# A fused attention and two-MLP kernel: early steps in another order on three engines, and the low parts of x on another engine

## The reference

```python
scores = where(causal, -1e9, q @ k.T / 8); a = softmax(scores)
local = a @ v
mem_out = (phi(q) @ M_prev) / (phi(q) @ z_prev + 1e-6)      # phi(x) = elu(x) + 1
x = g * mem_out + (1 - g) * local                           # g = sigmoid(beta), one per head
h = x @ w_in                                                # 2304 x 512 @ 512 x 1024
solu = h * softmax(h); ln = (solu - mu) / sqrt(var + 1e-6) * g_ln; x = ln @ w_out
return (sigmoid(x @ w_gate) * (x @ w_val)) @ w_out2         # 1536 wide
```

## Time and profile before

| | |
|---|---|
| median of 3 runs | 845.45 us |
| the profiled execution | 845.53 us |
| its span, first to last instruction | 843.5 us |
| PE busy over the span | 816.5 us, 97% |
| DVE, ACT, POOL busy | 601.1, 466.3, 39.0 us |
| mean granted TensorE clock | 0.995 of full |
| early steps (scores of step 1 to those of step 5) | 14.3 to 64.2 us |
| steps with the first MLP's tiles | 64.2 to 338.6 us |
| last tiles of the first MLP | 338.6 to 411 us |

### The profile page before, as it was taken

The page is one execution under the profiler, slowest core; times in us unless marked ns, Lnnn a source line. Parts: engine busy times, 40 slices in busy tenths (PEclk is TensorE's granted clock), DMA queues, the critical chain, the costliest instruction groups (busy, mean ns, idle before and its releaser), DMA issues.

```text
span 843.5 us, 15401 instructions
## 1 busy us (share of the span) xinstructions
PE 816.5 (97%) x5704; PEld 686.0 (81%) x5704; DVE 601.1 (71%) x1447; ACT 466.3 (55%) x965; POOL 39.0 (5%) x47
## 2 busy tenths in 40 slices
PE   5888999999999999999999999999999999999997
PEld 3555777777777777878889999999999999999996
DVE  6988877777777775588565777687676678666653
ACT  6987666666566663364444444574444465444442
POOL 1000000000000001111000000000000000000000
PEclk8999999999999999999999999999999999999999
DMA  7353011111111000100224111103111113111002
GB/s 219 91 171 88 18 53 54 53 54 54 47 44 54 26 18 15 51 1 1 75 54 148 51 51 51 51 26 125 50 51 51 51 27 125 51 51 50 26 1 76
DMA packets 67034, 49.51 MB, mean 59 GB/s; under 512 B 9360, under 2 KB 57488, under 8 KB 66960
## 3 DMA queue, kind: packets, MB, share of 16 engines
q1 hardware_dynamic: 66960, 48.53, 19.3%
HBM read 43.79 MB, written 4.72 MB: 58 GB/s over the span
## 4 chain that ended last, share of the span: by engine, by line
PE 90%; DVE 5%; issue 2%; ACT 2%; SPq 1%; DMA 1%; POOL 0%; DVEq 0%; ACTq 0%
PE tt_bk L1554 10%; PE tt_bk L1552 10%; PE tt_bk L1553 10%; PE m_bk L1420 10%; PE s_bk L1444 7%; PE tt_bk L1349 5%; PE s_bk L1290 4%; PE o_bk L1357 4%; PE o_bk L1444 4%; PE s_bk L1604 3%; PE s_bk L1605 3%; PE s_bk L1603 3%; PE m_bk L1604 2%; PE m_bk L1605 2%; PE m_bk L1603 2%
## 5 line engine op out<-in xcount | busy, mean ns | idle before, releaser
L1554 PE MATMUL tt_bk<-xc_hi,wc_lo 128*128 128x384 f32 x476 | 160.0, 336 | 0.0
L1552 PE MATMUL tt_bk<-xc_hi,wc_hi 128*128 128x384 f32 x476 | 159.9, 336 | 0.0
L1553 PE MATMUL tt_bk<-xc_lo,wc_hi 128*128 128x384 f32 x476 | 159.8, 336 | 0.0
L588 ACT ACTIVATE p_nat<-p_nat,negmax 128x512 f32<-128x512 f32 (+2 forms) x144 | 83.0, 579 | 53.3 <-DVE negmax L905 53.3
L1133 DVE TENSOR_TENSOR wc_lo<-wc_raw,wc_hi 128x768 fp32r<-128x768 f32 x72 | 78.3, 1088 | 32.0 <-ACT wc_hi L653 32.0
L1552 PEld LDWEIGHTS tt_bk<-xc_hi,wc_hi 128*128 128x128 f32 x476 | 89.4, 188 | 6.1
L1553 PEld LDWEIGHTS tt_bk<-xc_lo,wc_hi 128*128 128x128 f32 x476 | 89.4, 188 | 6.1
L1554 PEld LDWEIGHTS tt_bk<-xc_hi,wc_lo 128*128 128x128 f32 x476 | 89.4, 188 | 0.0
L905 DVE CUSTOM_DVE_ANT_0 p_nat<-s_bk,mask 128x384 f32<-128x384 f32 (+2 forms) x124 | 54.9, 489 | 19.4 <-PE s_bk L1290 18.9
L653 ACT CAST wc_hi<-wc_raw 128x768 fp32r<-128x768 f32 x72 | 64.5, 946 | 3.1 <-DVE wc_raw L1127 3.1
L1349 PE MATMUL tt_bk<-ident,p_nat 128*128 128x128 f32 x400 | 56.6, 277 | 7.6 <-ACT pT L595 7.4
(11 more groups left out here) (215 smaller groups left out, 1781.1 us busy)
## 6 DMA issues: line engine op xcount, KB each, us to landing
wc_raw<-in_moe_w_val SPq DMA_DIRECT2D x36, 256.0 KB, 3.0
wc_raw<-in_moe_w_gate SPq DMA_DIRECT2D x36, 256.0 KB, 3.4
qkT<-in_q SPq DMA_DIRECT2D x16, 288.0 KB, 2.8
qkT<-in_k SPq DMA_DIRECT2D x16, 288.0 KB, 3.2
v_raw<-in_v SPq DMA_DIRECT2D x16, 256.0 KB, 2.7
out<-o_sb SPq DMA_DIRECT2D x15, 256.0 KB, 2.5
w_raw<-in_moe_w_out SPq DMA_DIRECT2D x12, 256.0 KB, 4.5
turned<-in_k SPq DMA_DIRECT2D x32, 72.0 KB, 2.5
```

The source lines that it names most:

```text
L588: nc.scalar.activation(p_tile(g, tile), p_tile(g, tile), ACT.Exp, bias=negmax[:, n:n + 1], scale=-1.0, accum_out=den[:, n:n + 1]).then_inc ...
L1552: mm(o, hi[:, k, c, :], xc_hi[:, j, c, :], start=start and c == 0, stop=False, skip_group_check=True)
L1553: mm(o, hi[:, k, c, :], xc_lo[:, j, c, :], start=False, stop=False, skip_group_check=True)
L1554: last = mm(o, lo[:, k, c, :], xc_hi[:, j, c, :], start=False, stop=c == 1, skip_group_check=True)
```

## The change

Seven edits, all in the order of instructions but one.

1. Early steps, ScalarE: the copies of turned weights 0 to 2 stand ahead of exponential tile 2, and copies 3 to 6 ahead of tile 4; the copies of the values' result stand apart.
2. Early steps, VectorE: `normalize(g, 0)` stands right behind unit 3, `scale_memory(g - 1, 0)` behind unit 5, and `scale_memory(g - 1, 1)` with the split of the first weight behind unit 6, `feature` last.
3. Early steps, TensorE: `weighted` is two parts, the tail part behind `scores(g, 1)`; `memory` stands behind `turn_p(g - 1, 2)`.
4. Last pair's step (g = 16): TensorE transposes the MLP's tile ahead of the values and the output tile behind them; ScalarE has `moe_ln` ahead of `keep_both`; VectorE has `moe_ln_low` between two normalisations.
5. `split_x`, the low part of x, moves from GpSimd to VectorE for the tiles 0 to 12 but 4: tile 0 behind unit 3 of step 5, the others at the end of the step before theirs.
6. GpSimd keeps tile 4, the tiles from 13 on, and `rstd`.
7. Behind the steps: `moe_ln(12)` ahead of `moe_square(13)` on ScalarE, `moe_ln_low(12)` ahead of `moe_var(13)` on VectorE, with `low_xc(0, B21)` later.

```diff
 # GpSimd
-            def step(g):
-                if g >= M0:
-                    rstd(g - M0)
-                if g >= M0 - 1:
-                    split_x(g - M0 + 1)
...
+            def step(g, t):
+                if t and t in OWN:
+                    split_x(t)
+                rstd(t)
 # ScalarE, early_step
                 if g > 1:
-                    keep_both(g - 2)
+                    keep_x(g - 2, 0)
                 if g:
                     keep_pt(g - 1, 0)
+                if g > 1:
+                    keep_x(g - 2, 1)
+                if g:
                     keep_pt(g - 1, 1)
-                for n in range(2, 6):
+                    keep_pt(g - 1, 2)
+                exp_tile(g, 2)
+                exp_tile(g, 3)
+                if g:
+                    for n in range(3, NF):
+                        keep_pt(g - 1, n)
+                for n in range(4, 6):
                     exp_tile(g, n)
-                if g:
-                    keep_pt(g - 1, 2)
-                    keep_pt(g - 1, 3)
...
                 exp_tile(g, 6)
                 exp_tile(g, 7)
-                if g:
-                    keep_pt(g - 1, 4)
-                    keep_pt(g - 1, 5)
-                    keep_pt(g - 1, 6)
 # ScalarE, step
-                if t > 1 and g < PAIRS:
+                if t > 1:
                     moe_ln(t - 1)
                 keep_both(g - 2)
-                if t == 1 or g == PAIRS:
+                if t == 1:
                     moe_ln(t - 1)
 # ScalarE, behind the steps
             moe_y(t, True)
+            moe_ln(t + 1)
             moe_square(t + 2)
 # VectorE
+            def split_x(t):
+                dve.wait_ge(x_hi_ok, t + 1)
+                nc.vector.tensor_tensor(x_lo[:, :, :], xT[:, :, bass.ds(t * P, P)],
+                                        x_hi[:, :, :].bitcast(F32), ALU.subtract).then_inc(x_lo_ok, 1)
 # VectorE, early_step
                 unit_max(g, 2)
                 unit_max(g, 3)
+                normalize(g, 0)
+                unit_max(g, 4)
+                unit_max(g, 5)
                 if g:
                     scale_memory(g - 1, 0)
+                unit_max(g, 6)
+                if g:
                     scale_memory(g - 1, 1)
                     for c in W1_LO_MEM.get(g, ()):
                         split_w1(c)
-                unit_max(g, 4)
-                unit_max(g, 5)
                 feature(g)
...
-                unit_max(g, 6)
-                normalize(g, 0)
 # VectorE, step
-                if t > 1 and g < PAIRS:
+                if t:
                     moe_ln_low(t - 1)
...
-                if t == 1 or g == PAIRS:
-                    moe_ln_low(t - 1)
...
+                if t == 0:
+                    split_x(t)
...
                 moe_norm(t)
+                if t + 1 not in OWN:
+                    split_x(t + 1)
 # VectorE, behind the steps
-            low_xc(0, B21)
+            moe_ln_low(t + 1)
             moe_var(t + 2)
             moe_norm(t + 2, False)
+            low_xc(0, B21)
 # TensorE, early_step
                 if g > 1:
-                    weighted(g - 2)
+                    weighted_main(g - 2)
                 scores(g, 1)
+                if g > 1:
+                    weighted_tail(g - 2)
                 if g:
                     turn_p(g - 1, 0)
                     turn_p(g - 1, 1)
-                    memory(g - 1, None)
                 scores(g, 2)
                 if g:
-                    for n in range(2, 5):
-                        turn_p(g - 1, n)
+                    turn_p(g - 1, 2)
+                    memory(g - 1, None)
+                    turn_p(g - 1, 3)
+                    turn_p(g - 1, 4)
                 scores(g, 3)
 # TensorE, step
-                if g == PAIRS:
-                    pe.wait_ge(u_ok, t)
-                    weighted(g - 2)
-                if t > 1:
+                if 1 < t and g < PAIRS:
                     moe_out_t(t - 2)
...
-                if g < PAIRS:
-                    weighted(g - 2)
+                weighted(g - 2)
+                if g == PAIRS:
+                    moe_out_t(t - 2)
```

More of the change, by code:

```diff
@@ L551, in rstd @@
                 nc.gpsimd.tensor_tensor(st[:, 6:7], st[:, 5:6], half[:, :], ALU.pow).then_inc(rstd_ok, 1)
-            def step(g):
-                if g >= M0:
-                    rstd(g - M0)
-                if g >= M0 - 1:
-                    split_x(g - M0 + 1)
-            for g in range(PAIRS + 1):
-                step(g)
+            def step(g, t):
+                if t and t in OWN:
+                    split_x(t)
+                rstd(t)
+            for g in range(M0, PAIRS + 1):
+                step(g, g - M0)
             split_x(T_END + 2)
@@ L842, in _ @@
                 even = (i - t) % 2 == 1
-                moe_ln(i)
+                if i > t + 1:
+                    moe_ln(i)
                 if i == t + 1:
@@ L1238, in _ @@
             moe_stats(t + 2)
-            low_xc(0, B21)
+            moe_ln_low(t + 1)
             moe_var(t + 2)
             moe_norm(t + 2, False)
+            low_xc(0, B21)
             for i in range(t + 1, TILES):
                 even = (i - t) % 2 == 1
-                moe_ln_low(i)
+                if i > t + 1:
+                    moe_ln_low(i)
                 if i + 2 >= TILES:
@@ L1362, in turn_memory, with weighted_main @@
                    is_transpose=True, skip_group_check=True)
-            def weighted(h):
+            def weighted_main(h):
                 wait(pe, x_ok, 2 * h)
@@ L1381, in weighted, with weighted_tail @@
                 last.then_inc(o_ready, 1)
+            def weighted_tail(h):
                 for j in range(ST):
@@ L1385, in weighted @@
                 last.then_inc(o_ready, 1)
+            def weighted(h):
+                weighted_main(h)
+                weighted_tail(h)
             def memory(g, t):
```

## The result

| | before | changed |
|---|---|---|
| median | 845.45 us | 852.61 us (849.87 to 852.86) |
| the profiled execution's span | 843.5 us | 850.9 us |
| mean granted TensorE clock | 0.995 | 0.988 |

The ratio is 1.0074, with a 95% interval of 1.0063 to 1.0086: 6.3 us slower. The two medians lie 7.2 us apart, since the changed kernel's five times spread over 3 us and its median is near the upper end of them. In later rounds the same kernel took 850.03 us (median of four executions, 847.35 to 852.18), ratio 1.0055 (1.0034 to 1.0077).

The account below looks back on a forecast made before the run. TensorE was taken as full in steps 7 to 15 and the second MLP, so its waits elsewhere decide. +5.4 + 0.2 - 0.8 - 0.7 = +4.1 on 845.53, less 0.1, gave 849.5 us; own range 848.8 to 850.2, 8-in-10 range 845.3 to 851.8.

Parts of the forecast that it names:

- Up to `moe_hidden`: Early steps to the first tile's `moe_hidden`: start at about 78.1 us instead of 72.69, +5.4 with the slow clock.
- the piece: Last piece of `w1_lo` on VectorE in step 3: ends at 51.1 us instead of 48.25, bounds 48.1 and 52.4.
- Early steps on their own: Copies off TensorE's path: TensorE ready for scores 3 of pair 4 about 2.0 us earlier, at about 59.3.
- The transfer: Main term: late `w1_lo` delays the second weight and `turned`; scores 3 of pair 4 at 64.15, 2.85 us later.
- I take 3.0 of them: 51.1: VectorE, steps 1 to 3: 3.0 of its earlier 3.3 us of waits stay, so the `w1_lo` piece ends at 51.1.
- rival D: Step 1 slower too, by half clock: `w1_lo` piece ends at 52.4; 850.8 us, up to 851.8; chance 0.12.
- ScalarE's chain: Behind scores 3 of pair 4: 10.6 us of queued ScalarE work, then 0.85 for x_lo and handover before `moe_hidden`.
- The clock: Behind TensorE's 4.8 us wait for `turned`: half clock, +1.2 us, bounds 0 and 2.5.
- Step 6: TensorE waits for `ln_lo` before the memory part, as VectorE takes over the subtraction: +0.2 us.
- Step 16: Before the memory part: earlier transposing takes 0.8 of TensorE's 1.61 us idle time away, bounds 0 and 1.6.
- Behind the steps: The 0.70 us wait for `ln_lo` before `moe_out` of tile 12 disappears: -0.7, bounds 0 and 0.7.
- It goes wholly: The whole 0.70 us wait before `moe_out` at 367.05 goes, a tile of matmuls covering the work put behind it.

Follow-up runs that it names:

- e10: The changed kernel itself, unaltered, profiled a second time in later rounds; 850.03 us, ratio 1.0055.
- e1: The changed kernel with the last piece of `w1_lo` made early, behind unit 3 and ahead of `normalize(3, 0)`; 848.25 us, ratio 1.0024.
- e2: The changed kernel with the load of `turned` for pair 4 issued ahead of the second weight's DMAs; 847.10 us, ratio 1.0014.
- e5: The changed kernel with `turned` loaded ahead of the second weight and `w2_hi` pieces 2 to 4 behind `x_hi` of tile 0; 846.35 us, ratio 1.0009.
- e8: The changed kernel with only `w2_hi` pieces 2 to 4 taken behind `x_hi` of tile 0; 848.90 us, ratio 1.0042.
- e6: The kernel before with all of the change but the new order of the early steps; 843.31 us, ratio 0.9973.
- e3: The kernel before with the last piece of `w1_lo` moved late, behind unit 6 and `normalize(3, 0)` of step 3; 848.88 us, ratio 1.0039.
- e4: The kernel before with only the reorderings of the last pair's step and behind the steps; 844.69 us, ratio 0.9992.

## Why the prediction was right, and where it was off

Slower was forecast at 849.5 with a range to 851.8, and the median is 852.61; by the ratio it is 845.45 + 6.3 = 851.7, just inside, and by the later rounds 850.1. The mechanism held; sizes did not. Up to `moe_hidden` +5.4 was forecast and +7.26 measured. The 1.86 between them are: the piece 2.55 later than said, the way from the piece to the scores 0.59 shorter, the clock up to ScalarE's copy 0.17 cheaper, x_lo and its handover 0.07 longer.

*Early steps on their own.* TensorE was ready for scores 3 at 62.01 (66.11 - 4.10), not 59.3, and later than the 61.30 of before. At the end of step 1 TensorE was 0.7 us behind the kernel before; steps 2 and 3 are 0.4 us longer than before, not shorter. The waits for VectorE ahead of scores 2 came as forecast (1.38 to 1.39 us in steps 2 and 3). In e10, with full clock from 18 us on, it was ready at 60.5: 0.8 before the 61.30, not 2.0.

*The transfer.* The step that was mis-sized is "I take 3.0 of them: 51.1". VectorE waited 6.1 us, 4.0 of these in step 1, and the piece ended at 53.65, past my upper end of 52.4; in e10 at 52.13, within it. From there to the scores it took 12.46 us (13.05 forecast). The profile bore out rival D's cause, half clock in step 1.

*ScalarE's chain.* 10.60 us (10.6), x_lo and handover 0.92 (0.85): right. One reading in the sum was not: the 0.48 at 64.28, taken out as copy 4, is copy 6, of 128x384; copy 4 is the first of a pair that takes 1.06, so the sum is off by under 0.1. That TensorE idles for this chain even when the transfer is mended I had not said; e1 and e2 showed it. What it costs in time is not shown by itself: e5 and e8 took the wait away and lost as much behind it.

*The clock.* I took 1.2 us for the half clock behind the wait. It cost 1.03 up to ScalarE's copy (2.32 instead of 1.29 from scores 3 on), and then a third stretch in `moe_hidden`, 1.56 us, that I had not foreseen: the chain of ScalarE leaves TensorE idle a second time. It came in the first profile and not in e10, with all but the same waits. The rule of the Trainium skill cited in the prediction ("TensorE: Matmul & The Clock Gate", section "HAM oscillation") held behind the DMA wait, at 0.53.

*Step 6.* +0.21 (+0.2). VectorE's normalisation takes 1.14 us there again, with GpSimd's subtraction gone. *Step 16.* -0.61 (-0.8), TensorE's idle time 0.79 (0.8 forecast).

*Behind the steps.* The term "It goes wholly", -0.7, failed: the 0.70 at tile 12 is gone, and 0.94 stands at tile 13 (388.08), where before there was none. From step 16 to the second MLP nothing is won (+8.42 and, at the last matmul, +8.44). I had named no work that the moved instructions push back. That the result still lies in the range is luck: 1.0 us less came from the last stores, by no step of mine, and without it the 851.7 would be 852.7.

*Where the gain of the early order went.* From scores 0 of pair 2 to those of pair 5 e5, without any wait for `turned`, takes 38.71 us and e6, with the old order, 39.78: 1.07 faster. Step 4 gains 1.46 (11.92 against 13.38, and 11.92 in e2 too), steps 2 and 3 lose 0.39 (26.79 against 26.40). From there to `moe_hidden` it takes 9.67 against 8.02, and from there to step 6 20.46 against 18.99. So 1.07 is won and 3.1 given back, and 1.6 more by the clock behind it. (A part of the 3.1 is e5's own later `w2_hi`; e2, without that edit, takes 10.90 and 20.32, its half clock in `moe_hidden` included.) The copies were pulled ahead of ScalarE's exponentials and weights, but ScalarE's and VectorE's work up to `x_hi` is no less; TensorE's many waits of 1 us became a few of 2 to 4, and behind these the clock is half in many of the profiles.

Left open: how the other half of the loss divides between ScalarE's order, VectorE's and TensorE's, since VectorE's and TensorE's were not undone alone; and whether the new order itself makes the long half clock in step 1 likelier. It was there in 2 of 8 profiles with the new VectorE order (changed, e1; half clock over all of 18 to 22 us), and in none of 4 with the old.

## What to carry to other kernels

A moved instruction is priced by everything that waits for its semaphore, a DMA queue above all: here 1.2 us of subtraction, moved 5 us, held back 2 MB and the small tile behind them that had 0.13 us of slack. Where three engines have nearly equal loads, as here, an order that frees one of them can gather its waits in the place where the slowest must catch up. One long wait can cost more than three short ones, by the clock behind it: each of the six profiles with a wait of 3.2 to 4.8 us has half clock behind it (a mean of 0.50 to 0.62 over 64 to 68 us), and the waits of 1.16 us in the kernel before have none. When a wait is taken away, ask which work takes its place at the next tile.

## What the runs showed that I had not expected

The last stores. Landing times of the last DMAs (minimum, median, maximum in us), before, changed, and e6:

```profile
DMA to landing us min/median/max: 2.0/2.1/3.0
```

```profile
DMA to landing us min/median/max: 2.0/2.1/2.2
```

The first row is that of the kernel before, the second that of the changed kernel and of e6. In the kernel before and in e3 and e4 (3.1), in which GpSimd makes x_lo for all 18 tiles, one of the last stores takes 3.0 to 3.1 us; in the changed kernel and all eight others, with 12 of the tiles on VectorE, none takes over 2.2. This is the 1.0 us between last matmul and end (4.65 and 3.6), and it makes 1.0 of the 1.4 us by which e6 beats e4. Nothing here shows what these stores, 500 us behind the last moved subtraction (346.6 us in the changed kernel), have to do with it.

Half clock came with a delay: in the changed kernel `moe_hidden` started at full clock behind its 1.90 us of idling and fell to half 1.4 us later, while TensorE was working. In e5 it fell some 1.3 us after the work behind the 1.93 us had begun.
